# A fused attention and two-layer FFN kernel: moving one sum ahead of the upper gate and one copy ahead of the lower relu in the second layer

## The chip, the cores and the metric

The kernel runs on one core of one Trainium2 chip. The metric is device time in microseconds (us). One execution was also recorded by the profiler; every row below is from that one. TensorE (PE in the rows) multiplies, PEld is its weight load, VectorE is DVE, ScalarE is ACT, GpSimd is POOL, and SyncE (SP) issues the DMAs.

## What is computed

Pooled-key attention, then two feed-forward layers without biases over 4608 tokens of width 512 with 2048 hidden units:

```python
attn = softmax(q @ mean8(k).T / 8) @ mean8(v)   # 8 batches, 8 heads, 576 queries, 72 keys
x = attn.transpose(0, 2, 1, 3).reshape(4608, 512)
h = x @ w_in1;  x = maximum(0.01 * h, h) @ w_out1      # first layer
h = x @ w_in2;  x = (h * clip(h + 3, 0, 6) / 6) @ w_out2   # second layer
```

## The kernel before

**Tiles and steps.** A tile is 512 tokens. Tiles 0 to 8 are the first layer, tiles 9 to 17 the second. Attention for the next batch is woven into tiles 0 to 6; tiles 7 to 17 are feed-forward work alone. Each tile has 8 steps; step i makes an upper and a lower half of 128 hidden units each for all its tokens and multiplies the halves of the step before into the output. Every fp32 product is three products of rounded parts (high by high, high by low, low by high), so all factors exist as a `_hi` and a `_lo` buffer.

**Parts.** The 2 x 2 block product of a step is made with seven block products instead of eight (`part`, r = 0 to 6), each six matmuls of 256 columns into one of two PSUM banks. Between the parts TensorE does the output products of earlier steps (`second`, `pair_part`, `plain_half`). The engines put the blocks of h together from the banks: ScalarE copies the bank after part 1 of the seven to `p1` and after the third to c11 (a quarter of `h`); VectorE adds u2, u3, c22, c21 and, after the seventh, c12 (`h[:, 0, HN:N]`). c22 and c21 are the upper half, c11 and c12 the lower.

**Activation.** In the second layer `pre_of` (L1127, ScalarE) is the relu of h + 3, `gate_of` (L1398, VectorE) is min(pre, 6) * h and reads two SBUF buffers, `g_hi_of` (L1138, ScalarE) rounds it, `g_lo_of` (L1411, VectorE, two SBUF inputs) makes the rest. In the first layer the gate (L1392) needs no relu.

**Who waits for what on TensorE.** The first part of a step needs c12 of the step before (its bank is read by that sum); the second part needs c21; the third needs `p1`; the fourth u2; the fifth c11; the sixth u3; the seventh c22. From tile 11 on, step 1 of VectorE ends with four sums of the tile before's output (`y_of`, L1484: c22, y4, c12, c21 of y). In step 2, TensorE's first product that opens output bank S1 (`pair_part`, r = S1, i = 0 of the pair work) waits for the third of them.

**GpSimd.** Around step 1 of tiles 10 to 16 it makes four sums of the next tile's x (`t_sum`, L892 to L905), when the x loads land; around the last step it makes five remainders (`xs_lo`, L913). Both kinds read SBUF.

**Preparing w_in.** While the first layer runs, ScalarE, GpSimd and SP turn w_in of the second layer into seven block factors for each eighth: `factor2_hi` (L1083, ScalarE), `factors2_lo` (L934, GpSimd), `store_prep2` (L595, a DMA of SP). Four staging slots are shared, so the seventh factor waits until the third one's store has landed. Eighths 5 and 6 are made in tile 7 and eighth 7 in tile 8.

**Idle products.** `descend` (L1741) issues three matmuls of 256 columns into an unused half of a PSUM bank, with addresses that go down in steps of 16 elements. It runs in step 0 of tiles 7, 8 and 10 to 17 and in step 2 of tile 9, ahead of the fourth part.

**Order.** Each engine runs its instructions in the order written; nothing is rescheduled. `step` of ScalarE and VectorE and `pair_step` of TensorE are written out by place.

## Time and profile before

| | us |
|---|---|
| median of three timed runs | 1659.18 |
| lowest, highest | 1653.12, 1662.17 |
| the profiled execution | 1650.04 |
| its span, first to last instruction | 1648.2 |

The three timed runs differ by 9 us among themselves, and the profiled execution lies 3.1 us under the lowest of them. On the page, TensorE's share is a share of the span in which some matmul is in flight. Since matmuls overlap, their pace is read from the distance between their starts, or from how many lie in a stretch.

### The profile page before, as it was taken

What the parts mean: (1) busy time and instruction counts of PE and PEld (TensorE: products, weight loads), DVE (VectorE), ACT (ScalarE), POOL (GpSimd) and SP (SyncE); (2) the same over time, 40 slices, a digit from 0 to 9 for tenths busy, and PEclk for the clock granted to TensorE, in tenths of its full rate; (3) what the DMA queues carried; (4) which work ended last, traced back from release to release, by engine and by line L of the source; (5) the groups of instructions that cost most, each with busy time, mean ns of one, the idle gap of its engine ahead of it and who ended that gap; (6) DMA issues with size and microseconds to landing.
All of it is one profiled execution on the core that took longest, in us unless ns stands there. A gap on an engine that the chain in (4) does not pass through costs nothing.

```text
span 1648.2 us, 40178 instructions
## 1 busy us (share of the span) xinstructions
PE 1636.8 (99%) x13947; PEld 1614.8 (98%) x13947; DVE 1120.2 (68%) x2159; ACT 676.4 (41%) x1427; POOL 429.3 (26%) x451
## 2 busy tenths in 40 slices
PE   9999999999999999999999999999999999999998
PEld 8999999999999999999999999999999999999998
DVE  6768777686776867756455666676767676766665
ACT  5554443333332433333233444444444444444443
POOL 4346552021120212103335572030211111111100
PEclk9999999999999999999999999999999999999999
DMA  7746878778686786867789998898989898989894
GB/s 222 259 140 221 284 254 261 225 216 277 201 268 219 231 267 201 272 193 262 260 254 358 312 358 302 297 337 296 341 297 336 282 339 294 336 288 340 294 323 156
DMA packets 228572, 447.94 MB, mean 272 GB/s; under 512 B 23872, under 2 KB 48448, under 8 KB 219200
## 3 DMA queue, kind: packets, MB, share of 16 engines
q1 hardware_dynamic: 228416, 445.74, 80.9%
q8 instruction: 113, 1.85, 0.4%
q14 instruction: 43, 0.35, 0.1%
HBM read 379.58 MB, written 66.06 MB: 270 GB/s over the span
## 4 chain that ended last, share of the span: by engine, by line
PE 81%; DVE 2%; issue 1%; DMA 1%; ACT 0%; POOL 0%; DVEq 0%; ACTq 0%
PE ps_h L1804 36%; PE ps_y L1750 31%; PE ps_y L1891 5%; PE ps_att L1891 4%; PE ps_att L1928 2%; PE ps_att L1910 2%; PE ps_att L1729 1%; PE ps_att L1731 1%; PE ps_att L1730 1%; DMA w_in_split<-stage 1%; POOL stage L934 0%; DVE prob L1557 0%; PE ps_att L1741 0%; DVE h L1458 0%; DVE gate L1392 0%
## 5 line engine op out<-in xcount | busy, mean ns | idle before, releaser
L1804 PE MATMUL ps_h<-xs_hi,ring 128*128 128x256 f32 x3808 | 796.0, 280 | 1.8 <-DVE h L1458 0.8
L1804 PEld LDWEIGHTS ps_h<-xs_hi,ring 128*128 128x128 f32 x3808 | 635.9, 188 | 6.8 <-issue 3.6
L1804 PE MATMUL ps_h<-xs_lo,ring 128*128 128x256 f32 x1904 | 528.1, 277 | 0.0
L1804 PEld LDWEIGHTS ps_h<-xs_lo,ring 128*128 128x128 f32 x1904 | 358.6, 188 | 0.0
L1138 ACT ACTIVATE g_hi<-gate 128x512 fp32r<-128x512 f32 x288 | 182.1, 632 | 380.2 <-DVE gate L1392 200.6
L1750 PE MATMUL ps_y<-g_hi,wout_hi 128*128 128x256 f32 x1152 | 320.2, 278 | 0.6 <-DVE y_stage L1454 0.6
L1750 PE MATMUL ps_y<-g_hi,wout_lo 128*128 128x256 f32 x1152 | 319.2, 277 | 0.0
L1750 PE MATMUL ps_y<-g_lo,wout_hi 128*128 128x256 f32 x1152 | 319.1, 277 | 0.0
L1750 PEld LDWEIGHTS ps_y<-g_hi,wout_hi 128*128 128x128 f32 x1152 | 216.3, 188 | 1.2 <-DVE y_stage L1454 1.0
L1750 PEld LDWEIGHTS ps_y<-g_lo,wout_hi 128*128 128x128 f32 x1152 | 217.1, 188 | 0.0
L1750 PEld LDWEIGHTS ps_y<-g_hi,wout_lo 128*128 128x128 f32 x1152 | 216.3, 188 | 0.0
L1458 DVE TENSOR_TENSOR u<-ps_h,p 128x256 f32<-128x256 f32 x272 | 114.1, 419 | 124.0 <-PE ps_h L1804 104.7
L1127 ACT ACTIVATE pre<-h,three 128x512 f32<-128x512 f32 x144 | 103.2, 716 | 206.2 <-DVE h L1458 179.7
L1750 PE MATMUL ps_y<-wout_hi,g_hi 128*128 128x256 f32 x640 | 177.1, 277 | 0.0
L1750 PE MATMUL ps_y<-wout_lo,g_hi 128*128 128x256 f32 x640 | 177.1, 277 | 0.0
L1750 PE MATMUL ps_y<-wout_hi,g_lo 128*128 128x256 f32 x640 | 177.1, 277 | 0.0
L1398 DVE SCALAR_TENSOR_TENSOR gate<-pre,h 128x512 f32<-128x512 f32 x144 | 107.1, 744 | 67.2 <-ACT pre L1127 67.2
L1458 DVE TENSOR_TENSOR h<-ps_h,u 128x256 f32<-128x256 f32 x272 | 113.7, 418 | 54.6 <-PE ps_h L1804 53.0
L1407 DVE TENSOR_TENSOR g_lo<-gate,g_hi 128x512 fp32r<-128x512 f32 x144 | 109.8, 763 | 56.8 <-ACT g_hi L1138 56.6
L1411 DVE SCALAR_TENSOR_TENSOR g_lo<-gate,g_hi 128x512 fp32r<-128x512 f32 x144 | 105.6, 734 | 35.0 <-ACT g_hi L1138 34.9
L913 POOL TENSOR_TENSOR xs_lo<-x_stage,xs_hi 128x512 fp32r<-128x512 f32 x20 | 28.7, 1434 | 386.7 <-ACT xs_hi L1107 386.7
L1750 PEld LDWEIGHTS ps_y<-wout_lo,g_hi 128*128 128x128 f32 x640 | 120.3, 188 | 0.0
(155 smaller groups left out, 2862.1 us busy)
## 6 DMA issues: line engine op xcount, KB each, us to landing
ring<-w_in_split SPq DMA_DIRECT2D x920, 256.0 KB, 4.0
w_sums<-w_out_sums SPq DMA_DIRECT2D x64, 1024.0 KB, 6.2
w_in_split<-ring SPq DMA_DIRECT2D x56, 256.0 KB, 3.7
w_in_split<-stage SPq DMA_DIRECT2D x56, 256.0 KB, 3.9
k_raw<-in_kT SPq DMA_DIRECT2D x32, 288.0 KB, 4.0
q_raw<-in_qT SPq DMA_DIRECT2D x32, 288.0 KB, 5.3
v_raw<-in_v SPq DMA_DIRECT2D x32, 288.0 KB
x0T<-x_stage SPq DMA_DIRECT2D x32, 288.0 KB, 4.2
```

Source lines behind the costliest of these rows:

```text
L913: nc.gpsimd.tensor_tensor(xs_lo[second][:, r], x_block(r), xs_hi[second][:, r].bitcast(F32), ALU.subtract).then_inc(x_ready, 1 if r < NT4 ...
L1127: nc.scalar.activation(pre[:, upper], h[:, upper], ACT.Relu, bias=three[:]).then_inc(pre_ready, 1)
L1138: nc.scalar.activation(g_hi[layer == 2][:, g_slot(i, upper)], gate[:, upper], ACT.Copy, scale=1.0 / 6.0 if layer == 2 else 1.0).then_inc(g ...
L1398: nc.vector.scalar_tensor_tensor(gate[:, upper], pre[:, upper], 6.0, h[:, upper], ALU.min, ALU.mult).then_inc(gate_ready, 1)
L1407: nc.vector.tensor_tensor(g_lo[0][:, slot], gate[:, upper], g_hi[0][:, slot].bitcast(F32), ALU.subtract).then_inc(g_ready, 1)
L1411: nc.vector.scalar_tensor_tensor(g_lo[1][:, slot], gate[:, upper], 1.0 / 6.0, g_hi[1][:, slot].bitcast(F32), ALU.mult, ALU.subtract).then_ ...
L1458: return nc.vector.tensor_tensor(to, banks[bank], other, ALU.add)
L1750: mm = pe.matmul(bank[:, cols], left[a], right[b][:, cols], start=first and half == 0 and n == 0, stop=last and n == 2, skip_group_check=True)
L1804: mm = pe.matmul(banks[BANK_OF[r]], a, b[:, r, c, :], start=r in OPENS and c == 0 and n == 0, stop=c == 1 and n == 2, skip_group_check=True)
L1891: mm = pe.matmul(pair_banks[r], left[a], right[b], start=i == 0 and n == 0 and r in PAIR_OPENS, stop=i == HF - 1 and n == 2, skip_group_ch ...
L1910: mm = pe.matmul(u.ps[:, half, at * PAIR_KEYS:(at + 1) * PAIR_KEYS], q_of(b, c)[:, begins:begins + P], u.kT[:], start=True, stop=True)
L1928: mm = pe.transpose(at.ps[0:KEYS, hd, to:to + P - rows.start], u.prob[rows, SLOTS[half].start + 2 * j + hd, :], ident[rows, rows])
```

## The change

Four edits. (1) In the second layer VectorE makes c12 before the upper gate, not behind it. (2) In the second layer the lower relu leaves the end of its step and stands in the next step, behind the copy to `p1`. (3) In tiles 7 and 8 the seventh prepared factor of an eighth moves from place 6 of its last step to place 0 of the next (ScalarE), behind the `p1` copy and the lower `g_hi`, and SP's store of it to the first stream place of the next step. (4) `descend` is also called in step 5 of tile 17.

```diff
+LAST_STORES = tuple((2, r) for r in range(PRODUCTS - 1)) + ((3, 0),)
+LATE_PREP_AT = (0, 1, 2, 3, 4, 5, HF)
...
-                    if i in (2, 5):
+                    if i in (2, 5) and r < PRODUCTS - 1:
                         store_prep2(5 + i // 3, r)
+                    if i in (3, 6) and r == 0:
+                        store_prep2(4 + i // 3, PRODUCTS - 1)
...
-                    if i == 2:
-                        store_prep2(7, r)
+                    if (i, r) in LAST_STORES:
+                        store_prep2(7, LAST_STORES.index((i, r)))
...
-                        if 0 <= HF * i + m - begins < PRODUCTS:
-                            factor2_hi(eighth, HF * i + m - begins, T)
+                        at = HF * i + m - begins
+                        if not attention and at in LATE_PREP_AT:
+                            factor2_hi(eighth, LATE_PREP_AT.index(at), T)
+                        if attention and 0 <= at < PRODUCTS:
+                            factor2_hi(eighth, at, T)
...
                 nc.scalar.activation(p1[:], banks[0], ACT.Copy).then_inc(p1_ready, 1)
+                if (before if i == 0 else layer) == 2:
+                    pre_of(s - 1, 0)
...
-                    if m == 6 and layer == 2:
-                        pre_of(s, 0)
...
                 add(h[:, 1, 0:HN], 1, p1[:]).then_inc(c21_ready, 1)
-                gate_of(s, 1, layer)
+                if layer == 1:
+                    gate_of(s, 1, layer)
...
                 add(h[:, 0, HN:N], 0, u2[:]).then_inc(c12_ready, 1)
+                if layer == 2:
+                    gate_of(s, 1, layer)
...
-                if i == 0:
+                if i == 0 or T == ALL_TILES - 1 and i == 5:
                     descend(2)
```

On VectorE, step 1 of the looped second-layer tiles, before the change (`h<-ps_h,u` in the fourth row is c12, `gate<-pre,h` the upper gate, the rows behind `g_lo` are the sums of y, and `u<-ps_h,p` is u2 of step 2):

```order
L1458 TENSOR_TENSOR h<-ps_h,p 128x256 [waits product_done]
L1397 REGISTER_ALU [waits c22_ready,c21_ready,g_hi_ready,g_ready]
L1398 SCALAR_TENSOR_TENSOR gate<-pre,h 128x512 [waits pre_ready]
L1668 REGISTER_ALU
L1458 TENSOR_TENSOR h<-ps_h,u 128x256 [waits gate_ready,u2_ready,product_done]
L1405 REGISTER_ALU
L1411 SCALAR_TENSOR_TENSOR g_lo<-gate,g_hi 128x512 [waits g_hi_ready]
L1499 REGISTER_ALU
L1484 TENSOR_TENSOR y_stage<-ps_att,y 128x256 [waits y3_ready,gs_used]
L1484 TENSOR_TENSOR y<-ps_att,y 128x256
L1484 TENSOR_TENSOR y_stage<-ps_att,y 128x256 [waits y4_ready]
L1507 REGISTER_ALU
L1484 TENSOR_TENSOR y_stage<-ps_att,y 128x256 [waits g_used]
```

The same place after the change:

```order
L1467 TENSOR_TENSOR h<-ps_h,p 128x256 [waits product_done]
L1678 REGISTER_ALU
L1467 TENSOR_TENSOR h<-ps_h,u 128x256 [waits gate_ready,u2_ready,product_done]
L1406 REGISTER_ALU [waits c22_ready,c21_ready,g_hi_ready,g_ready]
L1407 SCALAR_TENSOR_TENSOR gate<-pre,h 128x512 [waits pre_ready]
L1414 REGISTER_ALU
L1420 SCALAR_TENSOR_TENSOR g_lo<-gate,g_hi 128x512 [waits g_hi_ready]
L1508 REGISTER_ALU
L1493 TENSOR_TENSOR y_stage<-ps_att,y 128x256 [waits y3_ready,gs_used]
L1493 TENSOR_TENSOR y<-ps_att,y 128x256
L1493 TENSOR_TENSOR y_stage<-ps_att,y 128x256 [waits y4_ready]
L1516 REGISTER_ALU
L1493 TENSOR_TENSOR y_stage<-ps_att,y 128x256 [waits g_used]
```

c12 now follows c21 (`h<-ps_h,p`) at once, and the gate has passed behind it; the rest of the row is as it was.

On ScalarE, at the boundary from step 0 to step 1 of a looped second-layer tile, before (`pre<-h,three` with c12 is the lower relu, `p<-ps_h` the copy to `p1`):

```order
L1138 ACTIVATE g_hi<-gate 128x512 [waits g_used]
L1127 ACTIVATE pre<-h,three 128x512 [waits gate_ready,c12_ready,c11_ready]
L1171 ISA
L1172 REGISTER_ALU [waits plain_bank]
L1173 ACTIVATE y_stage<-ps_y 128x512 [waits y_stored]
L458 REGISTER_ALU [waits pair_bank]
L1168 ACTIVATE y<-ps_y 128x256 [waits y_pair]
L1293 ISA
L1295 ACTIVATE p<-ps_h 128x256 [waits c21_ready,product_done]
L1133 REGISTER_ALU
L458 REGISTER_ALU [waits gate_ready]
L1138 ACTIVATE g_hi<-gate 128x512 [waits g_used]
```

After:

```order
L1143 ACTIVATE g_hi<-gate 128x512 [waits g_used]
L1176 ISA
L1177 REGISTER_ALU [waits plain_bank]
L1178 ACTIVATE y_stage<-ps_y 128x512 [waits y_stored]
L461 REGISTER_ALU [waits pair_bank]
L1173 ACTIVATE y<-ps_y 128x256 [waits y_pair]
L1301 ISA
L1303 ACTIVATE p<-ps_h 128x256 [waits c21_ready,product_done]
L1132 ACTIVATE pre<-h,three 128x512 [waits gate_ready,c12_ready,c11_ready]
L1138 REGISTER_ALU
L461 REGISTER_ALU [waits gate_ready]
L1143 ACTIVATE g_hi<-gate 128x512 [waits g_used]
```

The lower relu has passed behind the copy to `p1`, and it stands right ahead of the lower `g_hi`.

On ScalarE in tile 7, at the boundary from step 2 to step 3, before (`stage<-s_sum` is a prepared factor):

```order
L1138 ACTIVATE g_hi<-gate 128x512 [waits g_used,gate_ready]
L1083 ACTIVATE stage<-s_sum 128x256 [waits prep2_stored1,x_ready,s_summed]
L1083 ACTIVATE stage<-s_sum 128x256 [waits prep2_stored2,x_ready,s_summed]
L1295 ACTIVATE p<-ps_h 128x256 [waits c21_ready,product_done]
L1138 ACTIVATE g_hi<-gate 128x512 [waits g_used,gate_ready]
L1303 ACTIVATE h<-ps_h 128x256 [waits gate_ready,product_done]
```

After:

```order
L1143 ACTIVATE g_hi<-gate 128x512 [waits g_used,gate_ready]
L1088 ACTIVATE stage<-s_sum 128x256 [waits prep2_stored1,x_ready,s_summed]
L1303 ACTIVATE p<-ps_h 128x256 [waits c21_ready,product_done]
L1143 ACTIVATE g_hi<-gate 128x512 [waits g_used,gate_ready]
L1088 ACTIVATE stage<-s_sum 128x256 [waits prep2_stored2,x_ready,s_summed]
L1313 ACTIVATE h<-ps_h 128x256 [waits gate_ready,product_done]
```

The seventh factor, the one that waits for slot 2, has passed behind the copy to `p1` and the lower `g_hi`, and stands ahead of the c11 copy (`h<-ps_h`).

## Rows read from the trace of the kernel before

**Rows 1.** The page: busy time of the engines (part 1); the chain, by engine

```profile
PE 1636.8 (99%) x13947; PEld 1614.8 (98%) x13947; DVE 1120.2 (68%) x2159; ACT 676.4 (41%) x1427; POOL 429.3 (26%) x451
...
PE 81%; DVE 2%; issue 1%; DMA 1%; ACT 0%; POOL 0%; DVEq 0%; ACTq 0%
```

**Rows 2.** Stretches: us, then busy us (x instructions) of each engine, clock, DMA

```profile
1170.00:1230.00 60.00, 60.00 (x532) 60.00 (x531) 39.88 (x93) 24.37 (x45) 5.84 (x5) 1.00 0.92 322
1260.00:1315.00 55.00, 55.00 (x469) 55.00 (x468) 33.27 (x76) 22.69 (x41) 3.33 (x3) 1.00 0.88 303
1607.00:1640.00 33.00, 33.00 (x283) 33.00 (x282) 21.43 (x49) 12.64 (x23) 0.00 (x0) 1.00 0.47 163
```

**Rows 3.** Timeline of VectorE: start us, us, engine line op out<-in xcount [idle before]

```profile
1094.54 0.83 DVE L1398 SCALAR_TENSOR_TENSOR gate<-pre,h 128x512 f32<-128x512 f32 x1 [0.93 <-ACT pre L1127]
...
1153.69 1.17 DVE L1398 SCALAR_TENSOR_TENSOR gate<-pre,h 128x512 f32<-128x512 f32 x1 [0.93 <-ACT pre L1127]
...
1174.13 0.72 DVE L1398 SCALAR_TENSOR_TENSOR gate<-pre,h 128x512 f32<-128x512 f32 x1 [0.92 <-ACT pre L1127]
...
1175.63 0.92 DVE L1411 SCALAR_TENSOR_TENSOR g_lo<-gate,g_hi 128x512 fp32r<-128x512 f32 x1 [0.45 <-ACT g_hi L1138]
...
1177.26 0.76 DVE L1484 TENSOR_TENSOR y_stage<-ps_att,y 128x256 f32<-128x256 f32 x2
1177.93 0.41 DVE L1458 TENSOR_TENSOR u<-ps_h,p 128x256 f32<-128x256 f32 x1
...
1253.73 1.12 DVE L1398 SCALAR_TENSOR_TENSOR gate<-pre,h 128x512 f32<-128x512 f32 x1 [0.93 <-ACT pre L1127]
1254.78 0.41 DVE L1458 TENSOR_TENSOR h<-ps_h,u 128x256 f32<-128x256 f32 x1
...
1415.10 1.37 DVE L1398 SCALAR_TENSOR_TENSOR gate<-pre,h 128x512 f32<-128x512 f32 x1 [0.93 <-ACT pre L1127]
...
1604.54 0.69 DVE L1398 SCALAR_TENSOR_TENSOR gate<-pre,h 128x512 f32<-128x512 f32 x1 [1.25 <-ACT pre L1127]
```

**Rows 4.** Timeline of GpSimd around the same boundaries, columns as in group 3

```profile
1153.02 1.29 POOL L913 TENSOR_TENSOR xs_lo<-x_stage,xs_hi 128x512 fp32r<-128x512 f32 x1
1154.27 1.74 POOL L913 TENSOR_TENSOR xs_lo<-t_sum,xs_hi 128x512 fp32r<-128x512 f32 x1
...
1174.27 1.74 POOL L905 TENSOR_TENSOR t_sum<-x_stage,t_sum 128x512 f32<-128x512 f32 x1
...
1254.27 1.74 POOL L905 TENSOR_TENSOR t_sum<-x_stage,t_sum 128x512 f32<-128x512 f32 x1
```

**Rows 5.** Timeline of TensorE, tiles 7, 10 to 11, and 12

```profile
781.38 0.36 PE L1804 MATMUL ps_h<-xs_hi,ring 128*128 128x256 f32 x1 [0.55 <-ACT p L1295]
...
1155.09 0.28 PE L1891 MATMUL ps_y<-wout_hi,g_lo 128*128 128x256 f32 x1
1155.34 0.35 PE L1804 MATMUL ps_h<-xs_hi,ring 128*128 128x256 f32 x1
1155.53 0.28 PE L1804 MATMUL ps_h<-xs_lo,ring 128*128 128x256 f32 x1
...
1178.36 0.39 PE L1891 MATMUL ps_att<-w_sums,gs_hi 128*128 128x256 f32 x2
...
1180.40 0.28 PE L1804 MATMUL ps_h<-xs_hi,ring 128*128 128x256 f32 x1
...
1183.69 0.28 PE L1804 MATMUL ps_h<-xs_hi,ring 128*128 128x256 f32 x1
...
1185.50 0.28 PE L1804 MATMUL ps_h<-xs_hi,ring 128*128 128x256 f32 x1
```

**Rows 6.** Timeline of ScalarE, tiles 7 and 12

```profile
780.55 0.42 ACT L1083 ACTIVATE stage<-s_sum 128x256 fp32r<-128x256 f32 x1 [2.55 <-DMA w_in_split<-stage]
...
1176.52 0.39 ACT L1295 ACTIVATE p<-ps_h 128x256 f32<-128x256 f32 x1 [0.31 <-PE ps_h L1804]
...
1179.59 0.37 ACT L1303 ACTIVATE h<-ps_h 128x256 f32<-128x256 f32 x1
```

More of the change, by code:

```diff
@@ L1369, in _ @@
                 step(ALL_TILES - 1, i, 2, turns=False, pairs=True)
+            pre_of(HF * ALL_TILES - 1, 0)
             g_hi_of(HF * ALL_TILES - 1, HF - 1, 0, 2)
```

## The prediction

> **What bounds the kernel.** I read the page first: some matmul is in flight for 99% of the span, and TensorE is the chain [rows 1]. So the change adds or removes time only through what TensorE does: its starts held up, or its pace. The second needs counting, since busy time hides it. Instructions per stretch [rows 2] give 60.00 / 532 = 112.8 ns a matmul in tile 12, but 55.00 / 469 = 117.3 ns in tile 13 and 33.00 / 283 = 116.6 ns at the end of tile 17, all at a granted clock of 1.00, so it is no clock matter. I call these the low and the high pace. A pair step has 87 matmuls, so it takes 9.86 us at the low pace (TensorE's part at 1185.50 [rows 5], ten steps like it in that tile and the next) and 0.39 us more at the high one (87 x 4.5 ns). Following the starts through the second layer, the high pace begins at a held-up start and ends behind the next idle products. Of thirteen held-up starts from tile 7 on, at 780 us the first and at 1605 us the last, nine were followed by the high pace and four were not. What decides that, the trace does not show.
>
> Then the waits. At the boundary of tiles 10 and 11 the gate takes 1.17 us, where one without a neighbour takes 0.69 (the row at 1604.54) [rows 3]. GpSimd's remainder ends in it, and the next one takes 1.74 in place of 1.29 [rows 4]: the gate gets through between two GpSimd instructions, some 0.10 us before the second one's start. c12 stands behind the gate and comes late, and TensorE starts 0.25 us after its last start, not 0.11, and then 0.19 [rows 5]. Tile 13, step 1 to 2, is the same: gate 1.12, c12 from 1254.78 to 1255.19 [rows 3], step 2 at 1255.34.
>
> **The sum, part by part, against the profiled 1650.04 us.** (1.8 us lie outside its span.)
>
> *The prepared factor.* In tile 7 ScalarE waits 2.55 us for the landed store, then rounds, then copies p1, and TensorE stands idle 0.55 us [rows 5, 6]. Start to start that is 0.83 where 0.11 is due, 0.72 and 0.08 at the next start. Step 6 has the same at 812 us, worth 0.4. Behind the copy the factor's wait meets only the c11 copy, which tile 12 shows 0.81 us ahead of its user (1179.59 against 1180.40 [rows 5, 6]). SP's store passes one ring load that is wanted two steps later. Saved: 1.2.
>
> *Tile boundaries.* Seven, tiles 10 to 17 without 14 (at the high pace already). Each has 0.14 + 0.08 of held-up start and 3.3 us at the high pace until the idle products, 0.13: 0.35 each, and 0.45 for tile 10. With c12 ahead, it is ready as soon as the seventh part ends: 1183.69 + 0.28 [rows 5] leaves 1.53 us to the next step, 1.1 after an add of 0.41. The gate then asks about 0.34 us later than now. In this place GpSimd's change comes 0.48 us after the old asking (1.17 - 0.69), so the gate still gets it and ends when it does now, with 0.14 us to spare. Saved: 2.5.
>
> *Steps 1 to 2 of tiles 10, 13 and 15.* Held-up starts of 0.25, 0.18 and 0.43 (the gate took 1.37 in tile 15 [rows 3]). Saved: 0.9. With tile 13's goes its high pace, six steps and the start of tile 14: 6.1 x 0.39 = 2.4.
>
> *Tile 17.* The gate at 1604.54 was late without GpSimd, c12 came at 1605.6, 0.15 us ahead of step 5, and the high pace lasted to the end: some 325 matmuls x 4.5 ns = 1.5. With c12 ahead there is no hold-up. The three idle products cost 3 x 0.11 = 0.3 and then have nothing to mend. Saved: 1.2.
>
> Sum of the gains: 1.2 + 2.5 + 0.9 + 2.4 + 1.2 = 8.2 us.
>
> *What the later gate costs.* Here the choice lies. In step 1 GpSimd makes its four sums when the x loads land, so its changes fall differently in each tile. The gate's excess over 0.69 is how long it waited: in tiles 11 to 16 0.14, 0.03, 0.43, 0.15, 0.68, 0.03 (tiles 11, 12, 13 and 15 in [rows 3]; 14 and 16 repeat 11 and 12). Asking 0.34 us later, tiles 13 and 15 still catch the same change. Tiles 11, 12, 14 and 16 miss it: GpSimd has begun its next instruction (at 1174.27 in tile 12 [rows 4]) and holds for 1.26 us, so the gate ends 1.26 us later than now, at 1176.1 in tile 12. Behind it on VectorE are g_lo (via ScalarE's rounding) and the four sums of y. g_lo now takes 0.92 for a neighbour [rows 3]; in tile 12 that neighbour is gone by then and it takes 0.69, so the third sum of y, at 1177.68 now (the row at 1177.26 takes the third and the fourth together; the third has 0.42 of it), comes at 1178.7. TensorE's product of bank S1 is due at 1178.36 [rows 5] and starts at 1178.9: 0.5 held up, 0.1 at the next start. Then u2 (now 1177.93 [rows 3]), the lower gate and the c11 copy come about 1.0 late, and of the c11 copy's slack of 0.44 (1179.96 to 1180.40 [rows 5, 6]) less 0.15 for the semaphore, 0.25 is lost again. That is 0.85 for tiles 12 and 16. In 11 and 14 another GpSimd instruction is queued behind, g_lo meets it too, and the hold-up is 0.87 + 0.1 + 0.25 = 1.2. Tile 15 starts 0.4 earlier than now and loses 0.2 to its late sums. Costs: 2 x 0.85 + 2 x 1.2 + 0.2 = 4.3. Then the pace: from step 2 to the next idle products there are 5.7 steps, 2.2 us at the high pace. Bounds: none of the five tiles falls into it, 0; all do, 11. Nine of thirteen say 7.6; but a wait in the middle of a step is not shown, and there are two in each, so I take half, 2 tiles, 4.5.
>
> *The relu behind p1.* The p1 copy ends at 1176.91 [rows 6], the relu at about 1177.6, and u2 now ends at 1178.34 in that step, 1177.65 in one without sums of y: the lower gate is not later by over 0.05. At the other end, the p1 copy no longer stands behind a relu that the later g_hi would push 0.3 past it. Nothing either way. At the kernel's end the last gate is 0.3 late, 0 to 0.3.
>
> Net: -8.2 + 4.3 + 4.5 = +0.6, within 7.7 less and 7.1 more.
>
> **The Trainium skill against a row.** The rows of GpSimd and the gate [rows 3, 4] show that the two take turns and that a gate which asks first gets the next one. The Trainium skill says so too (SBUF — State Buffer, Who interferes with whom): whichever of the two issues first has the shared port pair for the whole instruction. It speaks against this change at step 1 and for its first half, since it lets an add that reads only one SBUF operand pass freely. Taken at its word, with the turn going to whoever issues first, it leaves open whether a gate that asks 0.14 us before the change at a tile boundary gets it; the rows show only gates that asked 0.48 us before. That case is in the second rival.
>
> **From the profiled execution to the median.** The profiled execution is 9.1 us under the median of the timed runs, more than the whole sum. The four together average 1656.1. The high pace can come to more tiles than the two seen, and stores can land later than in tile 7; both kernels are open to that, the changed one more in step 2 and less elsewhere. I set the forecast on the average: 1656.1 + 0.6, rounded down for tiles 7 and 8, where a hold-up can also start the high pace: **1656 us**, with 1651 to 1662 as its own range.
>
> **Rivals.** *The cover holds* (0.30). If the c12 add lets the gate ask earlier than I reckon, or GpSimd's sums fall after the gate in most tiles, the 4.3 and the 4.5 are gone: 1656 - 8 = 1648, and 1645 if the timed runs owed their extra time to the high pace. For it: all seven boundaries are alike to 0.02 us, so that gain is sure; against it: four of six tiles have the change of hands in just the 0.34 us that the gate now misses. *High pace in every tile* (0.09). Slower than before. S1 is held up in step 2 of each of tiles 11 to 16, each time followed by the high pace: 1656 + 6.6 = 1663, and if the gate also loses its 0.14 us to spare at the seven boundaries, where the p1 copy behind g_hi would then hold up the third part by some 0.2, up to 1668. It decides from four tiles on. *The added idle products do harm* (0.05). Called at the low pace in tile 17 they might start the high one: 0.3 + 4 steps x 0.39, 1658. In tile 8 they were issued at the low pace and left it low. *Nothing but noise* is inside the forecast (0.56).
>
> **Numbers.** 0.5%, about what a measurement of this kernel can tell from no change, is 8.3 us: faster is below 1650.9, slower above 1667.5. The first rival is nearly all faster (0.27) and the forecast's lower edge adds 0.05; the second is slower for 0.06 of its 0.09. Faster 0.32, same 0.62, slower 0.06. The range that leaves out two in ten: 1645 to 1664.
>
> **What would show it.** Right: no held-up start at tile boundaries and none in tile 7; c12 right behind c21, 1.1 us ahead of each step; gates of 1.2 to 1.9 us, or 0.69 ones asked late, in step 1 of some of tiles 11 to 16; gaps of 0.5 to 0.9 us at S1 in step 2 there, and fewer matmuls per us until the next idle products. Wrong: S1 on time in all tiles, or the pace low throughout the second layer.

## The result and the profile after

The changed kernel takes 1659.66 us (median of 20 runs) against 1653.34 us (20 runs of the kernel before); the ratio is 1.003, interval 1.0018 to 1.0042. It is slower by 0.3%: 4.9 us between the means, 6.3 between the medians. That is less than the 0.5% that the prediction names, but clear of noise, and it goes the other way than forecast: 1656 us was to be 3 us under the 1659.18 us known of the kernel before. On a second chip the ratio was 1.0023 (1.0006 to 1.0040), 4.6 us between the means.

The profiled execution took 1656.13 us, 6.1 us more than the one before. The page, TensorE and the chain (columns as in [rows 1]):

```profile
PE 1640.6 (99%) x13950; PEld 1618.6 (98%) x13950; DVE 1119.5 (68%) x2159; ACT 676.9 (41%) x1427; POOL 429.6 (26%) x451
PE 82%; DVE 1%; issue 1%; ACT 0%; DMA 0%; SPq 0%; POOL 0%; DVEq 0%; ACTq 0%; POOLq 0%
```

Neither line shows a loss of 6 us. What does is the length of each tile, from the first matmul of its first part to that of the next tile's (us):

| tile | before | after | after, second chip |
|---|---|---|---|
| 7 | 83.25 | 82.02 | 82.16 |
| 8 | 81.98 | 87.21 | 86.67 |
| 9 | 83.04 | 82.80 | 82.80 |
| 10 | 79.87 | 79.25 | 79.39 |
| 11 | 79.60 | 82.89 | 82.07 |
| 12 | 79.60 | 80.32 | 81.61 |
| 13 | 81.95 | 81.96 | 81.63 |
| 14 | 79.52 | 80.40 | 82.41 |
| 15 | 79.93 | 79.37 | 82.42 |
| 16 | 79.49 | 79.53 | 81.61 |
| 17, to the end | 87.91 | 87.21 | 87.34 |

Up to the start of tile 7 the changed kernel is 0.7 us ahead, by tiles that the change doesn't touch. Then tile 7 gives 1.2, tile 8 takes 5.2, and tiles 9 to 17 take 2.8: together 6.1.

**Tile 7** has all its steps from 1 on at 10.20 us. ScalarE (timeline, columns as in group 3 of the rows before) copies p1 with no store to wait for, and the last factor comes two places later; this answers [rows 5, 6]:

```profile
776.54 0.40 ACT L1088 ACTIVATE stage<-s_sum 128x256 fp32r<-128x256 f32 x1
778.80 0.38 ACT L1303 ACTIVATE p<-ps_h 128x256 f32<-128x256 f32 x1 [1.86 <-PE ps_h L1817]
780.54 0.63 ACT L1143 ACTIVATE g_hi<-gate 128x512 fp32r<-128x512 f32 x1 [1.35 <-DVE gate L1401]
781.08 0.40 ACT L1088 ACTIVATE stage<-s_sum 128x256 fp32r<-128x256 f32 x1
```

**Tile 8.** TensorE stands still in step 4, and its first matmuls behind that are 213 ns apart (the timeline of TensorE, then the stretches, columns PE busy, clock, DMA share, GB/s):

```profile
872.02 0.28 PE L1763 MATMUL ps_y<-g_hi,wout_lo 128*128 128x256 f32 x1
875.09 0.55 PE L1817 MATMUL ps_h<-xs_hi,ring 128*128 128x256 f32 x1 [2.79 <-ACT p L1303]
...
876.51 0.41 PE L1763 MATMUL ps_y<-g_hi,wout_hi 128*128 128x256 f32 x1
876.72 0.41 PE L1763 MATMUL ps_y<-g_lo,wout_hi 128*128 128x256 f32 x1
...
860.00:870.00 10.00, 10.00 (x91) 1.00 0.90 315
870.00:880.00 10.00, 7.21 (x52) 0.83 0.53 177
880.00:890.00 10.00, 10.00 (x88) 1.00 1.05 388
```

There are three losses in one place. 3.07 us lie between two starts where 0.11 is due, and 0.35 before the next: 3.2 lost. Then the granted clock is 0.83 in the slice: eleven matmuls at 213 ns, the lower of the two levels, lose 1.1. Then 88 matmuls in 10 us in place of 90 is the high pace, some 190 matmuls long, 0.9. That is the 5.2.

What TensorE waited for is found by following the waits back from the p1 copy: ScalarE, GpSimd, SP. First the kernel before, then the changed one:

```profile
873.20 0.36 ACT L1295 ACTIVATE p<-ps_h 128x256 f32<-128x256 f32 x1
...
868.51 0.74 POOL L947 TENSOR_TENSOR out_sum<-out_raw 128x256 f32<-128x256 f32 x1 [5.43 <-DMA w_in_split<-stage]
```
```profile
873.35 1.33 ACT L1159 ACTIVATE w_sums<-out_sum 128x256 fp32r<-128x256 f32 x4 [4.54 <-POOL out_sum L957]
874.59 0.36 ACT L1303 ACTIVATE p<-ps_h 128x256 f32<-128x256 f32 x1
...
863.53 0.94 POOL L939 TENSOR_TENSOR stage<-s_sum,stage 128x256 fp32r<-128x256 f32 x1 [3.17 <-ACT stage L1088]
870.39 0.74 POOL L952 TENSOR_TENSOR out_sum<-out_raw 128x256 f32<-128x256 f32 x1 [5.92 <-issue]
...
861.35 3.09 SPq L517 DMA_DIRECT2D x_stage<-x1T  x4
864.49 0.43 SPq L566 DMA_DIRECT2D ring<-w_in_split  x1
864.96 0.43 SPq L598 DMA_DIRECT2D w_in_split<-stage  x1
```

In tile 8, unlike tile 7, three more things hang on the last store of the eighth. GpSimd waits for it to land (`stores2_done`) before it makes the sums of w_out, and by the trace it landed 0.2 us ahead of the first of them; ScalarE rounds those sums in step 3, ahead of the p1 copy of step 4; and SP loads the next tile's x at the end of step 2, so that the moved store now stands behind four loads of 256 KB. The p1 copy, at 873.20 in a tile that began at 830.85 before, is at 874.59 in one that began at 828.92: 3.3 us later.

**Second layer.** Of the seven boundaries from 10 to 11 up to 16 to 17, six have no held-up start, 10 to 11 has one at its third part (0.46 us). The boundary of tiles 11 and 12 answers [rows 3]: c12 first, the gate behind it without a wait.

```profile
1159.51 0.42 DVE L1467 TENSOR_TENSOR h<-ps_h,u 128x256 f32<-128x256 f32 x1 [0.99 <-PE ps_h L1817]
1159.85 0.68 DVE L1407 SCALAR_TENSOR_TENSOR gate<-pre,h 128x512 f32<-128x512 f32 x1
```

In step 1 of tile 12 the gate asks 0.10 us after GpSimd's change, and everything behind it is late:

```profile
1180.04 1.29 POOL L910 TENSOR_TENSOR t_sum<-x_stage,t_sum 128x512 f32<-128x512 f32 x1
...
1180.14 1.74 DVE L1407 SCALAR_TENSOR_TENSOR gate<-pre,h 128x512 f32<-128x512 f32 x1
1182.66 0.69 DVE L1420 SCALAR_TENSOR_TENSOR g_lo<-gate,g_hi 128x512 fp32r<-128x512 f32 x1 [0.78 <-ACT g_hi L1143]
...
1184.05 0.76 DVE L1493 TENSOR_TENSOR y_stage<-ps_att,y 128x256 f32<-128x256 f32 x2
...
1184.53 0.50 PE L1904 MATMUL ps_att<-w_sums,gs_hi 128*128 128x256 f32 x2 [0.34 <-DVE y_stage L1493]
...
1186.38 0.36 ACT L1313 ACTIVATE h<-ps_h 128x256 f32<-128x256 f32 x1
...
1186.89 0.36 PE L1817 MATMUL ps_h<-xs_hi,ring 128*128 128x256 f32 x1
```

The product of S1 starts 0.51 us late and its second matmul another 0.11; the fifth part (1186.89, behind c11) 0.13 and 0.08. The pace, in stretches of 40 us of tiles 11, 12 and 13 of this execution, then of tiles 12 and 16 of the second chip's:

```profile
1112.00:1152.00 40.00, 40.00 (x342) 1.00 0.85 298
1194.00:1234.00 40.00, 40.00 (x355) 1.00 0.91 312
1274.00:1314.00 40.00, 40.00 (x342) 1.00 0.88 303
```
```profile
1193.00:1233.00 40.00, 40.00 (x342) 1.00 0.85 301
1521.00:1561.00 40.00, 40.00 (x342) 1.00 0.87 303
```

342 is the high pace, 355 the low one, both at a granted clock of 1.00. The first execution has two tiles of it (11 and 13), the second all six from 11 to 16, so it took 1664.27 us in place of 1656.13. Tile 17's end stays at the low pace, 267 matmuls in 30 us against [rows 2]:

```profile
1615.00:1645.00 30.00, 30.00 (x267) 30.00 (x267) 19.35 (x47) 11.94 (x22) 0.00 (x0) 1.00 0.47 165
```

### The profile page after: what moved, and what is told of

Its sections match the earlier page's. It is cut to its first block, busy times and chain, and to the rows that moved or that the text cites. A ratio compares the mean times of both kernels' runs of the same rounds, so it can differ in the third digit from the quotient of the medians.

```text
span 1654.3 us, 40190 instructions
## 1 busy us (share of the span) xinstructions
PE 1640.6 (99%) x13950; PEld 1618.6 (98%) x13950; DVE 1119.5 (68%) x2159; ACT 676.9 (41%) x1427; POOL 429.6 (26%) x451
## 3 DMA queue, kind: packets, MB, share of 16 engines
q8 instruction: 113, 1.85, 0.4%
## 4 chain that ended last, share of the span: by engine, by line
PE 82%; DVE 1%; issue 1%; ACT 0%; DMA 0%; SPq 0%; POOL 0%; DVEq 0%; ACTq 0%; POOLq 0%
PE ps_h L1817 37%; PE ps_y L1763 31%; PE ps_y L1904 5%; PE ps_att L1904 4%; PE ps_att L1941 2%; PE ps_att L1923 2%; PE ps_att L1742 1%; PE ps_att L1744 1%; PE ps_att L1743 1%; DVE gate L1407 0%; DMA w_in_split<-stage 0%; PE ps_att L1754 0%; SPq L517 0%; DVE xs_lo L1434 0%; ACT g_hi L1143 0%
## 5 line engine op out<-in xcount | busy, mean ns | idle before, releaser
L1763 PEld LDWEIGHTS ps_y<-wout_hi,g_hi 128*128 128x128 f32 x640 | 120.3, 188 | 0.0
L1763 PEld LDWEIGHTS ps_y<-wout_hi,g_lo 128*128 128x128 f32 x640 | 120.3, 188 | 0.0
```

Of the source, the lines that this page charges most:

```text
L1763: mm = pe.matmul(bank[:, cols], left[a], right[b][:, cols], start=first and half == 0 and n == 0, stop=last and n == 2, skip_group_check=True)
```

## The experiments

All ratios are to the kernel before on the same chip; the versions under one heading below ran on one chip, `edge3b` and `e_edge` on another. "Mean" is the difference of the means in us (uncertain by about 1 us), "dev." the standard deviation of the kernel's own 12 runs in us (of before 2.7 to 3.9). "High" are the tiles 10 to 16 whose profile is at the high pace in step 4.

| kernel | ratio (interval) | mean | dev. | tile 8 | high |
|---|---|---|---|---|---|
| e_prep | 0.9993 (0.9975-1.0010) | +0.2 | 3.1 | 86.30 | 12, 13 |
| e_layer2 | 0.9993 (0.9973-1.0013) | -0.8 | 3.7 | 82.11 | none |
| e_prep7 | 0.9985 (0.9966-1.0003) | -2.2 | 3.1 | 81.98 | 15, 16 |
| e_keep1 | 0.9992 (0.9972-1.0013) | -0.5 | 3.8 | 83.42 | 10, 16 |
| after2 | 1.0023 (1.0006-1.0040) | +4.6 | 3.6 | 86.67 | 11 to 16 |
| e_no8 | 1.0001 (0.9983-1.0018) | +1.5 | 3.6 | 83.81 | 11, 12, 13, 15, 16 |
| e_sum8 | 0.9999 (0.9982-1.0016) | -0.5 | 2.3 | 83.80 | 10, 12, 16 |
| e_st8 | 1.0018 (0.9998-1.0037) | +2.5 | 3.3 | 84.74 | none |
| e_idle3 | 0.9994 (0.9979-1.0009) | -1.0 | 1.5 | 81.98 | none |
| e_best1 | 0.9998 (0.9980-1.0016) | +0.3 | 2.8 | 83.42 | 14 |
| e_best2 | 0.9995 (0.9977-1.0013) | -1.3 | 1.8 | 82.31 | none |
| e_relu | 0.9998 (0.9982-1.0015) | -0.2 | 2.2 | 83.93 | 13 |
| layer2b | 1.0004 (0.9983-1.0024) | +1.5 | 5.1 | 84.76 | 13 to 16 |
| e_c12 | 1.0029 (1.0012-1.0046) | +4.4 | 2.3 | 82.11 | 10, 11, 12, 15 |
| e_idle3n | 0.9987 (0.9973-1.0001) | -2.0 | 1.5 | 84.27 | none |
| e_edge3 | 0.9971 (0.9955-0.9987) | -4.0 | 2.8 | 82.30 | none |
| edge3b | 0.9973 (0.9961-0.9985) | -4.2 | 1.3 | 83.83 | none |
| e_edge | 0.9973 (0.9958-0.9988) | -4.2 | 3.6 | 81.98 | 16 |

### The parts one by one

`e_prep` is the prepared-factor edit alone, `e_layer2` the other three edits, `e_prep7` is `e_prep` without its half in tile 8 (here and below a diff is against the version named beside it, and `late_gate` is true where the gate stands behind c12):

```diff
-                    if (i, r) in LAST_STORES:
-                        store_prep2(7, LAST_STORES.index((i, r)))
+                    if i == 2:
+                        store_prep2(7, r)
...
-                        late = isinstance(T, int) and T in (7, 8)
+                        late = isinstance(T, int) and T in (7,)
```

`e_keep1` is `e_layer2` with the gate where it was in step 1 alone:

```diff
-                late_gate = layer == 2 and (True)
+                late_gate = layer == 2 and (not (i == 1 and pairs_before))
```

> The kernel before with the prepared-factor edit alone (stores and sums of eighths 5 to 7 one place on; gate, relu and idle products as before). Theory A, the store: in tile 8 SP's last store of eighth 7 stands behind the loads of the next tile's x, GpSimd waits for its landing, ScalarE waits for GpSimd's sums ahead of the p1 copy, and TensorE stands still for 3 us in step 4; tile 8 takes 87 us in place of 82 and the ratio is 1.002 (+3.3 us, 5.2 lost in tile 8 less 1.9 gained in tile 7). Rival B, the layer-2 order is what costs and tile 8 of the changed kernel was one odd execution: tile 8 takes 82 us, tile 7 is 1.2 to 1.9 shorter, ratio 0.999.

> The changed kernel without the prepared-factor edit: c12 ahead of the upper gate, p1 copy ahead of the relu, three more idle products. Theory A: what these three cost in the profile of the changed kernel, tiles 9 to 17, is +2.8 us (gains at boundaries and in tile 17 of 2 to 3, losses of 5 to 6 at S1 in step 2 and by the high pace behind it); ratio 1.001 to 1.002, and held-up S1 products in step 2 of tiles 11, 12, 13, 14. Rival C, the pace falls by chance: the tiles at the high pace differ from those of the changed kernel, and the ratio lies within 0.001 of 1.

> The prepared-factor edit for eighths 5 and 6 alone (tile 7), the rest as before. Theory A: no held-up start in steps 3 and 6 of tile 7, all steps of it 10.20 us, tile 8 as before at 82 us: -1.2 to -1.9 us, ratio 0.999. Rival: the stores one ring load later land later too, GpSimd's sums come too late as in tile 8, and a held-up start stays in step 4: ratio 1.000.

> As the changed kernel without the prepared-factor edit, but in step 1 of the tiles with sums of y the upper gate stays ahead of the c12 add. Theory B, the later gate in step 1 holds up S1 of step 2 and the high pace follows: here S1 starts within 0.1 us of its nominal time in step 2, the tiles 11, 12, 14 go back to 79.6 us or less, boundaries stay clean: -3 to -5 us against before, ratio 0.997 to 0.998. Rival C, the high pace comes by chance and not from S1: tiles at the high pace turn up all the same, ratio 0.999 to 1.001. The step 1 to 2 hold-ups of 0.2 to 0.4 us in tiles 10, 13 and 15 come back in either case.

The traces bear out theory A: tile 8 is 86.30 us with the edit and 81.98 without its tile 8 half, tile 7 is 82.2 in both, with no held-up start. The timed runs didn't: `e_prep` has a ratio of 0.9993 where 1.002 was expected, and the intervals, 0.0018 to each side, are as wide as the effect. The two together (+0.2 against -2.2 in the mean) have the right sign and half the size. `e_layer2` missed its 1.001 to 1.002 too, and its profile has no tile at the high pace. Of theory B in `e_keep1` the hold-ups came true: S1 and the fifth part start on time in step 2 of all tiles 11 to 16. Its gain of 3 to 5 us did not come (-0.5), and tiles 10 and 16 were at the high pace, tile 10 from a held-up seventh part of step 1 and tile 16 from a held-up start of step 2, where the old order still holds up c12.

### Tile 8: the late sum or the late store

`after2` is the changed kernel again and `e_no8` the changed kernel with tile 8 as before. `e_sum8` and `e_st8` are `e_prep7` with one half each of tile 8's edit: the last factor sum two places later, with its store at the old place in SP's queue, or the store alone behind the x loads.

```diff
e_sum8:
-                        late = isinstance(T, int) and T in (7,)
+                        late = isinstance(T, int) and T in (7, 8)
...
e_st8:
-                    if i == 2:
-                        store_prep2(7, r)
+                    if (i, r) in LAST_STORES:
+                        store_prep2(7, LAST_STORES.index((i, r)))
```

> The changed kernel itself, on the chip on which its parts are timed. Its prepared-factor edit alone gave a ratio of 0.9993 and its layer-2 edits alone 0.9993. If the parts add up, this one lies at 0.999 +- 0.003 here; if the first measurement (1.003) holds here too, some 5 us come from the parts together, and its trace should show a stall that neither part shows. In either case: tile 8 at 86 to 87 us with TensorE idle for 3 us in step 4, held-up S1 products in step 2 of three to six tiles of the second layer.

> The changed kernel with eighth 7 (tile 8) prepared as before; eighths 5 and 6 one place on, and the layer-2 edits as changed. Theory A (tile 8's stall is the main cost): tile 8 at 82 us (84.5 if the high pace comes), and 4 to 5 us less than the changed kernel on the same chip, ratio to the changed kernel 0.997. Rival B (the layer-2 order is the main cost): within 1 to 2 us of the changed kernel.

> The kernel before with the prepared-factor edit for eighths 5 and 6, and in tile 8 the last factor sum two places later (behind the p1 copy of the next step), but its store at its old place in SP's queue, ahead of the x loads. Theory A1, the late sum is what makes the store late: the sum ends 3 us later against the start of the tile than before, GpSimd's sums of w_out follow it, TensorE idles 2.5 to 3 us in step 4, tile 8 86 us. Theory A2, the x loads ahead of the store do it: the store lands at most 1 us later than before and tile 8 stays at 82 to 83 us. Here SP also waits in front of its x loads: they go out 1 to 2 us later.

> The counterpart: factor sums of tile 8 at their old places, only the last store moved behind the x loads and one ring load. Theory A1: the store is issued when SP has done the x loads, 3 to 4 us after the sum, so part of the delay comes back by this way: landing 3 us later than before and 1 to 2 us of idle TensorE in step 4, tile 8 84 us; if the late sum alone is to blame, tile 8 stays at 82 us. Theory A2: the whole 3 us, tile 8 86 us.

`after2` is as slow as in the first measurement (+4.6), though its two groups of edits had given +0.2 and -0.8 alone, and its trace has no stall that neither of them shows; that the times of the parts do not add up stays open. `e_no8` against `after2`, same chip: 3.1 us less in the mean (expected 4 to 5). So tile 8 looks like the larger part of the 4.6, not by a margin that the times alone would prove. The other two decide between the halves, because they issue the store at the same moment of the tile (35.57 and 35.67 us from its start). SP and GpSimd of `e_sum8`, then of `e_st8`:

```profile
864.42 0.33 SPq L598 DMA_DIRECT2D w_in_split<-stage  x1
864.86 1.81 SPq L517 DMA_DIRECT2D x_stage<-x1T  x4
...
866.66 0.74 POOL L952 TENSOR_TENSOR out_sum<-out_raw 128x256 f32<-128x256 f32 x1 [2.27 <-issue]
```
```profile
862.19 2.90 SPq L517 DMA_DIRECT2D x_stage<-x1T  x4
865.13 0.43 SPq L566 DMA_DIRECT2D ring<-w_in_split  x1
865.61 0.43 SPq L598 DMA_DIRECT2D w_in_split<-stage  x1
...
871.05 0.73 POOL L952 TENSOR_TENSOR out_sum<-out_raw 128x256 f32<-128x256 f32 x1 [7.99 <-DMA w_in_split<-stage]
...
875.76 0.36 PE L1817 MATMUL ps_h<-xs_hi,ring 128*128 128x256 f32 x1 [2.45 <-ACT p L1304]
```

From the store's issue to GpSimd's next sum it is 2.2 us with the x loads behind it and 5.4 with four of them and one ring load ahead of it. 5 x 256 KB at the 358 GB/s that the stretch from 860 to 870 us of `e_st8` moved are 3.7 us. The store lands 37.61 us into the tile in `e_sum8`, though issued 3.2 us later than before, where it landed at 37.45; in `e_st8` it lands at 40.90. TensorE idles 2.6 us in `e_st8` and 0.23 in `e_sum8`. Theory A2 holds: the place in the DMA queue did it, and A1 falls. Its sizes were off: tile 8 took 84.74 in `e_st8` where 86 was expected, since there neither the clock fell nor the high pace came, and 83.80 in `e_sum8` where 82 to 83 was. The late sum has no part in that 83.80: eight traces with tile 8 as before have the same start held up by 0.23 to 0.45 us, six of them with the high pace behind it, and a ninth (`layer2b`) by 1.05. The late sum costs nothing, since SP waits for it while the queue ahead drains. (The Trainium skill, DMA: Bandwidth & Descriptors, Issuing engines are not separate DMA queues, says that all these transfers run on the same 16 DMA engines and interleave, so a second issuing engine would not have helped by bandwidth; no run here tried one.)

That is why one pair of profiles puts tile 8 too high. The three with the whole edit average 86.7 us there, the fifteen with tile 8 as before 82.9 (81.98 to 84.76): 3.8 us, near the 3.1 of the timed runs.

The timed runs fit in another way. The mean granted clock of a run is below 1.000 in 49 of 56 executions of the four kernels with the store behind the x loads, and in 78 of 180 of the other changed ones.

### The pace: what ends it, and what starts it

From tile 10 on, every stretch at the high pace in the traces ends at idle products, at another held-up start or with the kernel. `e_idle3` is `e_no8` with three more idle products in step 3 of each tile from 10 on:

```diff
-                if i == 0 or T == ALL_TILES - 1 and i == 5:
+                if i in (0, 3) or T == ALL_TILES - 1 and i == 5:
                     descend(2)
```

`e_best1` is `e_keep1` with the tile 7 edit, `e_best2` the same with these idle products, and `e_relu` moves the relu behind p1 in the kernel before, and nothing else.

> The changed kernel with tile 8 as before (as in the run that showed five tiles of the second layer at the high pace), and three more idle products ahead of the fourth part in step 3 of each tile 10 to 17: 8 x 0.33 = 2.6 us more. Theory P (the high pace begins at a held-up start and any idle products end it): high pace may begin at the fourth part's hold-up of step 2, but ends in step 3; no tile from 11 to 16 over 80.9 us, the layer at 79.3 + 0.33 + up to 0.8 a tile, and 1 to 5 us less than its counterpart in the median, ratio to before 0.998 to 1.000. Rival: the idle products only end it at the boundary of a tile, or start it as often as they end it: tiles of 82 to 83 us remain, ratio 1.001 to 1.002.

> Put together from what cost nothing: eighths 5 and 6 one place on, eighth 7 as before, c12 ahead of the upper gate in every step of the second layer but step 1 of the tiles with sums of y, p1 ahead of the relu, the idle products of tile 17. If the parts add up (means against before -2.2 and -0.5 us): -2.7 us, ratio 0.998; S1 of step 2 on time, no tile end held up, tile 7 and 8 at 82.0. Rival: nothing but the scatter of the high pace, 1.000.

> The same with three idle products also in step 3 of tiles 10 to 17 (2.6 us more). Theory P: the two high-paced tiles of a usual execution (2 x 2.3 us) shrink to 0.8 us each, so in the mean it is 0.4 us faster or equal, but its scatter is smaller: executions within 1646 to 1652. Rival: 2.6 us slower at the same scatter.

> The kernel before with the p1 copy ahead of the lower relu alone. Forecast: nothing either way, ratio 1.000 +- 0.002; starts at tile boundaries 0.14 + 0.08 us late as before, tile 7 with its 0.55 us gap. Rival: the relu one place later makes the lower gate and the c11 copy late, and TensorE's fifth part of a step (192 ns gaps as in the changed kernel) is held up without any change to the gate: then part of the high pace comes from here, ratio 1.001.

The second half of theory P holds: idle products end the high pace. In `e_idle3` four tiles (10, 11, 13, 16) entered the high pace in steps 1 and 2 and none kept it; tile 13 on both sides of its idle products at 1268.5:

```profile
1260.00:1268.00 8.00, 8.00 (x70) 1.00 1.00 359
1270.00:1310.00 40.00, 40.00 (x355) 1.00 0.86 293
```

Two of the matmuls counted in a stretch lap over its edges, so it is 8.00 / 68 = 117.6 ns ahead of them and 40.00 / 353 = 113.3 behind. The scatter of the time falls from 3.6 us (`e_no8`) to 1.5, and it is 1.8, 1.5, 2.8 and 1.3 in the other four measurements with these idle products against 2.2 to 5.1 without them. So the scatter of this kernel from execution to execution is for the most part the number of tiles at the high pace. The idle products pay for their 2.6 us where there are many such tiles and are even where there are few: `e_idle3` is 2.5 us under `e_no8` (on another chip), `e_best2` 1.6 under `e_best1`, and below `edge3b` equals `e_edge`. The executions of `e_best2` lie at 1645.5 to 1652.1, 1646 to 1652 expected. `e_best1` missed its 0.998: the parts' gains of -2.2 and -0.5 were within their own error. `e_relu` came out as forecast: no difference in time, and its tile starts are held up by 0.13 us as before.

The first half, that the high pace begins at a held-up start, is the rule with exceptions. In tile 14 of `e_best1` it begins at a start of step 2 that is 0.02 us late over three matmuls, and at the start of step 1 of tile 9 it begins in every trace with no hold-up. Ahead of tile 10 it also ends without help: in step 6 of tile 8 in three traces, the changed kernel's among them.

### What the later gate costs

`layer2b` repeats `e_layer2` on another chip. `e_c12` is edit 1 alone. `e_idle3n` is the kernel before with the tile 7 edit and the idle products of step 3, and `e_edge3` adds edit 2 and, in the last step of each tile alone, edit 1 (the gate's line of the diff):

```diff
-                late_gate = layer == 2 and (False)
+                late_gate = layer == 2 and (i == HF - 1)
```

> The layer-2 edits alone, a second time, on another chip. Theory L (the later gate starts the high pace in 3 of 6 tiles): mean 2 to 3 us over before, some tiles of the profile at 81.6 to 82.4 us whose high pace begins at the fifth part (part 4) of step 2. Rival (chance, no cost): within 1 us of before, as the first time.

> c12 ahead of the upper gate alone; relu, idle products and prepared factors as before. Theory L: as the layer-2 edits together, or 1.2 us more for tile 17's end: 2 to 4 us over before, the fifth part of step 2 held up by 0.1 to 0.2 us in most of tiles 11 to 16, S1 by 0.2 to 0.6 in two or three. Rival: same as before; or the hold-up of the fifth part is gone, since here the lower relu stands where it stood: then the relu's move is what makes c11 late.

> The kernel before with eighths 5 and 6 one place on and three idle products in step 3 of tiles 10 to 17, no layer-2 edit. Scatter small (standard deviation 1.5 us, as with the same idle products above). Tile boundaries held up by 0.14 + 0.08 us each. Against the version with the layer-2 edits and the same idle products (mean 1.0 us under before): theory L, whose cost is taken away here with the high pace cut short, predicts 0 to 1 us more than that one, mean 0 to 1 us under before; if the layer-2 edits cost by themselves, 1 to 3 us less than that one.

> The same, but the upper gate behind c12 in the last step of each tile alone, and the p1 copy ahead of the relu. It takes the boundary gain (7 x 0.35 us) without the cost in step 2: 1.5 to 2.5 us less than its neighbour in this call, no held-up tile starts (one at tile 10 to 11 may stay, where part 3 waits for p1), S1 and the fifth part of step 2 on time. Mean 2 to 3 us under before, ratio 0.998.

The hold-ups are settled by counting in all traces (late is the first or the second matmul of the part). In the seven profiles of a kernel with the gate behind c12 in step 1, the fifth part of step 2 is held up in all 42 tiles 11 to 16, by 0.08 to 0.18 us, and the product of S1 by over 0.05 in 23 of them, up to 0.55. In the other thirteen neither is held up in any of 78 tiles (0.02 us at most). Behind that, without idle products in step 3, the high pace holds in 20 of 36 tiles against 11 of 54: 3.3 tiles of an execution against 1.2. At 2.3 us a tile that would be 4.8 us for the order of two instructions in one step. This count is not as sure as the first: tiles of one execution are not independent, and the same kernel had none (`e_layer2`) and four (`layer2b`). Nor do the timed runs prove it: the four measurements with the gate late in step 1, tile 8 as before and no idle products in step 3 are at -0.8, +1.5, +1.5 and +4.4 us. `layer2b` was expected at 2 to 3.

`e_c12` is as slow as the whole change (+4.4) without touching tile 7 or 8. In it the third part of step 1 is held up in tiles 11 to 16 as well (0.08 us), and by 0.77 in step 0 of tile 11: the p1 copy stands behind a relu that the later g_hi pushes. The rival, that the relu's move makes c11 late, falls: the fifth part is held up without it.

`e_idle3n` was to tell whether the later gate costs by the high pace alone. It is 1.0 us under `e_idle3` (on another chip), where theory L said 0 to 1 over and the other reading 1 to 3 under: the hold-ups of the layer-2 edits seem to cost by themselves, within an error as large.

`e_edge3` against `e_idle3n`, same chip, is 2.0 us less (uncertain by 0.9): the boundary gain, 1.5 to 2.5 expected. The last two runs put it to another chip, with and without the idle products:

> Repeat of the version that measured 0.9971, on another chip. If its gain is its own and not the chip's: mean 3 to 4 us under before, ratio 0.9975 +- 0.001, the standard deviation 1.5 to 2.8 us against 3.5 of before. If it was chance: 0.999 or more.

> The same without the idle products in step 3: the boundary gain of 2.5 us and tile 7's 1.2 us stay, 2.6 us of idle products are saved, but the high pace runs on to the end of the tile again in 1 to 2 tiles of an execution (2.3 us each). Expected 0 to 1.5 us slower in the mean than its neighbour, standard deviation back at 3 us or more, ratio 0.998 to 0.999.

The repeat gave 0.9973 again, with a deviation of 1.3 us. `e_edge` gave the same mean (-4.2, interval of the ratio 0.9958 to 0.9988) with a deviation of 3.6; I had given it up to 1.5 us more. Its profile in tiles 12 and 16:

```profile
1187.00:1227.00 40.00, 40.00 (x355) 1.00 0.92 309
1505.00:1545.00 40.00, 40.00 (x342) 1.00 0.89 294
```

Both are under both kernels: 0.27% under before, with intervals that leave out 1, and by the ratios 0.5 to 0.6% under the changed one. They consist of the tile 7 half of edit 3, edit 2, and edit 1 at tile boundaries.

## Why the prediction was wrong, point by point

**The prepared factor.** This step failed, by what it left out. For tile 7 it was right: forecast 1.2, measured 1.2 in the profile (over all traces 82.1 us with the edit and 84.2 without). For tile 8 it had no term. "SP's store passes one ring load that is wanted two steps later" is true in tile 7; in tile 8 the store passes four x loads too, and GpSimd, ScalarE and the p1 copy hang on it. The term is +5.2 in the profile, +3.8 over all traces, +3.1 in the mean of timed runs: with the +5.2 the forecast of +0.6 against the profile of before would have been +5.8, where 6.1 was measured. The trace of before had it: GpSimd took up the sums of w_out only when that store had landed, ScalarE rounded them right ahead of p1 (873.20, 42.35 us into the tile), and there was 0.4 us to spare, since in `e_sum8` the copy comes at 42.94 and TensorE idles 0.23. A store 3 us later could only end in an idle TensorE.

**Tile boundaries.** Right in mechanism and nearly in size. No start at the first part is held up, the gate asks 0.3 to 0.35 us later against the step (0.34 forecast), and takes 0.68 to 0.82 at six of the seven. At 10 to 11 it asks 0.94 us ahead of the step, not 1.16 to 1.23, and misses GpSimd's change: 1.85 us, and p1 behind it holds up the third part by 0.46 and 0.08. The prediction took all boundaries for alike; why the ask is later there stays open. Nor were the gains alike: "3.3 us at the high pace" does not follow the starts of tiles 15 and 16 of the kernel before (113.6 ns a matmul), so 2.3 was due there in place of 2.5, and of the thirteen held-up starts seven, not nine, were followed by the high pace. `e_edge3` against `e_idle3n` measures the whole at 2.0.

**Steps 1 to 2, and tile 13.** The starts of step 2 are on time, as forecast. The high pace of tile 13, 2.4 us, came back all the same: it now begins at the fifth part, 5.2 us into the step.

**Tile 17.** Forecast 1.2, measured 0.7, of which 0.2 are the start of the tile and belong to the boundaries: the high pace is gone, and held-up starts of 0.06 and 0.34 us near the end, where the last products wait for `gs`, took some back.

**The later gate.** The mechanism was right, its places and its size were not. 4.3 was forecast for the hold-ups, S1 by 0.5 in tiles 11, 12, 14 and 16 and then 0.25 at the fifth part. The trace has S1 late by 0.14, 0.51, 0.16 and 0.16 in tiles 11 to 14 and the fifth part in all six (0.08 to 0.17); with the 0.08 to 0.11 at each next matmul they make 2.7. Two more hold-ups bring it to 4.0, but not by the term forecast: the seventh part of step 1 by 0.30 and 0.33 in tiles 11 and 14, which I had not seen and which stands ahead of the later gate (`e_best1` and `e_prep` have it too), and the third part of tile 11. That the sum comes near 4.3 is luck. Where GpSimd's change falls in a tile moved with the tile's start, so single tiles could not be forecast.

**The high pace behind it.** 2 tiles and 4.5 us were forecast, and the profile has 2 tiles, 11 and 13. Over five profiles of the layer-2 edits without idle products it is 3.4. The rival *high pace in every tile*, given 0.09, is what the second profile of the changed kernel shows: 1664.27 us, against the 1663 worked out for it. The nearness of the two is luck: S1 was late in two of its six tiles only, the fifth part did the rest, and 4.7 us are tile 8's. As a median it did not come.

**The relu behind p1.** "Nothing either way" holds alone (`e_relu`, 0.9998) but not beside edit 1: without it (`e_c12`) edit 1 holds up the third part in each step 1 of tiles 11 to 16. The prediction had named that end.

**The cover holds** fell: that rival needed GpSimd's sums to fall behind the gate in most tiles, and even where they did, the fifth part was late.

**From the profile to the median.** I set the forecast on the mean of the four times shown, 1656.1. Over 20 runs the kernel before has 1653.3. On that base the same sum would be 1654, and with the missing 3 to 5 us of tile 8 it would be 1657 to 1659, just under the measured 1659.7. So the base was 3 us too high and the sum 4 to 6 us too low, and that the measured time lies inside the stated range is luck. (The "7.7 less" of the prediction is not worked out: the gains alone are 8.2, and with the hold-ups 3.9.)

## What to carry to other kernels

When a DMA moves past others in a queue, price it in each place of the loop on its own: list what is queued ahead of it there and who waits for its landing, since the same edit gained 1.2 us in one tile and lost 5.2 in the next. When a wait is taken from the critical engine by letting another instruction go late, look for the step in which that second chain has no slack, and make the exchange only in the steps where it pays: at the boundary alone, with the tile 7 edit, it was worth 0.3%; everywhere, it gave no such gain, and alone (`e_c12`) it cost 0.3%. Where executions scatter by as much as the effect, find what scatters, count it in each trace, and measure with it suppressed.

## What the runs showed of the hardware

- TensorE has two paces at one granted clock of 1.00: 113.3 and 117.8 ns between the starts of 256-column matmuls. A held-up start of as little as 0.08 us can switch it either way (it began at one in tile 11 of `after2` and ended at one, the second matmul of S1, in tile 14), and from tile 10 on the next three idle matmuls ended the high one in every case where it lasted until them. The Trainium skill (TensorE: Matmul & The Clock Gate, Back-to-back issue gap) gives, for an isolated matmul at the high clock, columns over 2.4 GHz plus 2.5 ns, an estimate of 109.2 ns for 256 columns; both levels measured here lie above it, and the measurement decides. What sets the two levels is not settled.
- An idle time of 3.0 us of TensorE was followed by matmuls at 213 ns, the lower clock level, in both profiles of the changed kernel, 11 and 16 matmuls long. 2.58 us in `e_prep` was too, 1.6 us after the restart; 2.61 us in `e_st8` was not, with a granted clock of 1.00 throughout.
- From the issue of one 256 KB store to the instruction that waited for its landing it was 2.2 us with one ring load still under way (it landed 1.1 us after the issue, `e_sum8`) and 5.4 us behind five more transfers of the same size (`e_st8`).
- In the changed kernel a VectorE gate that reads two SBUF buffers took 0.68 us with no GpSimd instruction near (step 1 of tile 17), 0.82 when it asked 0.23 us ahead of the start of GpSimd's next instruction (boundary of tiles 12 and 13), and 1.74 when it asked 0.10 us behind that start (step 1 of tile 12).
